# Routing tables, start-up loads and code placement in a fused attention and two-layer mixture-of-experts kernel

## The reference

```python
def _attn_ref(r, k, v, w, u):            # batch 4, 8 heads, 768 steps, head size 48
    for t in range(S):
        kt, vt, rt = k[:, :, t], v[:, :, t], r[:, :, t]
        cur = einsum('bhd,bhe->bhde', u[None] * kt, vt)
        y[:, :, t] = einsum('bhd,bhde->bhe', rt, state + cur)
        state = w[None, :, :, None] * state + einsum('bhd,bhe->bhde', kt, vt)

def _moe_ref(x, w_skip, w_gate, w1, w2): # 3072 rows of 384, 8 experts, hidden size 1024
    do = x @ w_skip > 0
    e, gate = argmax(x @ w_gate), its softmax value
    return x + where(do, gate * (relu(x @ w1[e]) @ w2[e]), 0)

def _moe2_ref(x, w_gate, w1, w2):        # the same without skip and residual
    return gate * (relu(x @ w1[e]) @ w2[e])
```

## Time and profile before

| | us |
|---|---|
| median of 3 runs | 594.66 (594.61 to 594.92) |
| the profiled execution's own time | 589.84 |
| its span | 588.1 |
| TensorE busy | 539.8 (92%) |
| VectorE busy | 387.9 (66%) |
| ScalarE busy | 251.9 (43%) |
| GpSimd busy | 249.9 (42%) |
| mean granted TensorE clock | 0.971 |

### The profile page before, as it was taken

How to read it: one execution, slowest core, us unless ns; L and a number is a source line. 1 busy time by engine, 2 the same in 40 slices (tenths; PEclk the granted TensorE clock), 3 DMA queues, 4 the chain that set the end, 5 groups by cost and what they waited for, 6 DMA issues and landing times. The chain is left out here.

```text
span 588.1 us, 16050 instructions
## 1 busy us (share of the span) xinstructions
PE 539.8 (92%) x5550; PEld 512.8 (87%) x5551; DVE 387.9 (66%) x839; ACT 251.9 (43%) x704; POOL 249.9 (42%) x348
## 2 busy tenths in 40 slices
PE   3999999988799999999857879999999999999992
PEld 3899998978699999999855769999999999999992
DVE  5888888867688878888613927463747464647330
ACT  0233333334077667776413017362736352626220
POOL 5887778742244444454410043232534323324331
PEclk9999999997899999999969989999999999999997
DMA  9798888876187777776378014544444534111100
GB/s 140 121 188 165 161 161 162 169 254 224 43 312 223 209 230 250 244 236 212 60 245 304 0 54 115 185 157 147 139 165 153 162 140 147 50 46 43 39 15 26
DMA packets 114127, 89.58 MB, mean 152 GB/s; under 512 B 80672, under 2 KB 104931, under 8 KB 114080
## 3 DMA queue, kind: packets, MB, share of 16 engines
q1 hardware_dynamic: 106304, 74.16, 45.1%
q0 software_dynamic: 7776, 14.82, 9.1%
HBM read 80.44 MB, written 13.27 MB: 159 GB/s over the span
## 5 line engine op out<-in xcount | busy, mean ns | idle before, releaser
L822 DVE TENSOR_TENSOR w_lo<-w_raw,w_hi 128x384 fp32r<-128x384 f32 (+1 forms) x224 | 130.2, 608 | 4.7 <-ACT w_hi L817 3.1
L1092 PE MATMUL e_ps_h<-e_x_hi,w_hi 128*128 128x192 f32 (+3 forms) x384 | 119.6, 311 | 3.2 <-DVE e_x_lo L1210 2.9
L817 ACT CAST w_hi<-w_raw 128x384 fp32r<-128x384 f32 (+1 forms) x224 | 119.9, 566 | 3.8 <-issue 3.5
L1094 PE MATMUL e_ps_h<-e_x_hi,w_lo 128*128 128x192 f32 (+3 forms) x384 | 119.6, 311 | 0.0
L1093 PE MATMUL e_ps_h<-e_x_lo,w_hi 128*128 128x192 f32 (+3 forms) x384 | 119.5, 311 | 0.0
L1250 DVE SCALAR_TENSOR_TENSOR e_h_lo<-e_ps_h,e_h_hi 128x128 fp32r<-128x128 f32 (+1 forms) x192 | 70.5, 396 | 44.5 <-ACT e_h_hi L1179 40.1
L1092 PE MATMUL e_ps_y<-w_hi,e_h_hi 128*128 128x384 f32 x272 | 95.5, 351 | 0.0
L1094 PE MATMUL e_ps_y<-w_hi,e_h_lo 128*128 128x384 f32 x272 | 91.5, 336 | 0.0
L1093 PE MATMUL e_ps_y<-w_lo,e_h_hi 128*128 128x384 f32 x272 | 91.1, 335 | 0.0
L1092 PEld LDWEIGHTS e_ps_h<-e_x_hi,w_hi 128*128 128x128 f32 x384 | 72.9, 190 | 5.4 <-DVE e_x_lo L1210 3.4
L1094 PEld LDWEIGHTS e_ps_h<-e_x_hi,w_lo 128*128 128x128 f32 x384 | 72.9, 190 | 1.2
(11 more groups left out here) (168 smaller groups left out, 922.4 us busy)
## 6 DMA issues: line engine op xcount, KB each, us to landing
w_raw<-in_moe_w_dram SPq DMA_DIRECT2D x32, 1536.0 KB, 7.3
r_in<-in_r_dram SPq DMA_DIRECT2D x24, 192.0 KB, 3.2
k_in<-in_k_dram SPq DMA_DIRECT2D x24, 192.0 KB, 3.9
v_in<-in_v_dram SPq DMA_DIRECT2D x24, 192.0 KB, 4.0
x_rows<-rows SPq DMA_DIRECT2D x24, 192.0 KB, 3.5
w_lo<-x_rows SPq DMA_DIRECT2D x6, 768.0 KB, 6.6
x_in<-x_rows,e_ent_in POOLq DMA_INDIRECT x33, 3.1
out_dram<-y_rows,e_ent_out POOLq DMA_INDIRECT x19
```

Of the source, the lines that this page charges most:

```text
L817: act.copy(self._of(self.hi1[par], self.hi2[par], n), self._of(self.raw1[par], self.raw2[par], n)).then_inc(self.hi_done[par], 1)
L822: eng.tensor_tensor(self._of(self.lo1[par], self.lo2[par], n), self._of(self.raw1[par], self.raw2[par], n), self._of(self.hi1[par], self.h ...
L1092: pe.matmul(o, s_hi, m_hi, start=(k == 0), stop=False)
L1094: return pe.matmul(o, s_lo, m_hi, start=False, stop=(k == last))
```

## The change

1. Attention's head: w is loaded straight into `w_pow[:, 0]`, by ScalarE's queue, as is u; VectorE waits for w alone. SP begins with r and k at once. GpSimd zeroes only the padding columns. `shrink` is no longer a reciprocal: GpSimd builds it in a ladder of seven multiplies while VectorE builds `grow`. `shrink_up` is made after the first `rk`, and turned by TensorE after the scores of step 0. Loads of r, k and of v get semaphores of their own.
2. Routing: the place is split into row and column in float; instead of 14 wide VectorE instructions there are, for each of the 24 tiles, one for `col_hot` (38 or 45 columns, ids only) and one for `row_hot` (128 columns), both with per-partition scalars, so the placing product has half the columns and its result is copied by one instruction.
3. Experts' head: 24 `gate_hot` instructions on VectorE, 24 products `row_hot` x `gate_hot` on TensorE ahead of `stay_warm`, which has two turns instead of three, and a copy to `gates`; the m = 0 pieces of W.lo come behind that copy.
4. `load_rows` starts two DMAs of half the size.
5. For m = 1, ScalarE's and VectorE's routing programs stand in a one-trip loop whose head is placed at slot 0 of a block of 256 instructions.
6. The wait for the last scatter of m = 1 goes from GpSimd to SP. A smaller edit: the iota that the chain needs has its own semaphore.

```diff
 # attention: SP, GpSimd, ScalarE, VectorE, TensorE
-            sp.wait_ge(dve_zeroed, 2)
-            for j in range(2):
-                sp.dma_start(w_col[PAD * j:PAD * j + D, :], ...).then_inc(small, 16)
-            sp.dma_start(u_row[:], ...).then_inc(small, 16)
...
-                pool.memset(r_in[n][:], 0.0).then_inc(zeroed, 1)
-                pool.memset(k_in[n][:], 0.0).then_inc(zeroed, 1)
+                pool.memset(r_in[n][:, :, D:PAD], 0.0).then_inc(zeroed, 1)
+                pool.memset(k_in[n][:, :, D:PAD], 0.0).then_inc(zeroed, 1)
...
+            pool.memset(shrink[:, :, HALF - 1:HALF], 1.0).then_inc(shrunk, 1)
+            for n in range(6):
+                m = 2 ** n
+                pool.wait_ge(shrunk, n + 1)
+                pool.wait_ge(tables, POWERS[n])
+                pool.tensor_tensor(shrink[:, :, HALF - 2 * m:HALF - m], shrink[:, :, HALF - m:HALF], w_pow[:, n, :]..., ALU.mult).then_inc(shrunk, 1)
+            pool.wait_ge(shrunk, 7)
+            pool.wait_ge(tables, LOW)
+            pool.tensor_tensor(shrink[:, :, HALF:P], shrink[:, :, 0:HALF], grow[:, :, 0:1]..., ALU.mult).then_inc(shrunk, 1)
...
+            act.wait_ge(dve_zeroed, 1)
+            for j in range(2):
+                act.dma_start(w_pow[PAD * j:PAD * j + D, 0, :], ...).then_inc(w_loaded, 16)
+            act.dma_start(u_row[:], ...).then_inc(u_loaded, 16)
...
-            dve.wait_ge(small, 48)
-            link(dve.tensor_copy(w_pow[:, 0, :], w_col[:]))
+            dve.wait_ge(w_loaded, 32)
...
-            link(dve.reciprocal(shrink[:, :, 0:P // 2], grow[:, :, 1:P // 2 + 1]))
-            link(dve.tensor_tensor(shrink[:, :, P // 2:P], ...))
-            link(dve.tensor_tensor(shrink_up[:], ...))
...
+            dve.wait_ge(shrunk, 8)
             rk(0, 0)
+            dve.tensor_tensor(shrink_up[:], ...).then_inc(tables, 1)
...
-                pe.wait_ge(loaded[b], 48 * (c + sub // 4 + 1))
+                pe.wait_ge(rk_loaded[b], 32 * (c + sub // 4 + 1))
...
                 ins.then_inc(scored, 1)
+                if isinstance(i, int) and i == 0:
+                    pe.wait_ge(tables, TABLE_STEPS + 1)
+                    for p in range(NP):
+                        ins = pe.transpose(ps_x[:, P * p:P * p + P], shrink_up[:, p, :], ident[:])
+                    ins.then_inc(tab_ps, 1)
...
                 wait(pe, state_done, i)
+                pe.wait_ge(v_loaded[b], 16 * (c0 + sub0 // 4 + 1))
                 pe.wait_ge(k_end_done, i + 1)
 # load_rows
-    eng.dma_start(dst, x_rows.rearrange(...)[g]).then_inc(x_loaded[g], 16)
+    for n in range(2):
+        eng.dma_start(dst[:, half * n:half * n + half, :], src[:, half * n:half * n + half, :]).then_inc(x_loaded[2 * g + n], 16)
 # route
+        def from_line_start(eng):
+            return nc.Fori(0, 1, engines=[eng.engine], head_slot={eng.engine: 0}) if TURN else nullcontext()
...
-            dve.wait_ge(made, 7)
+                dve.wait_ge(e_made, 1)
...
-            link(dve.tensor_scalar(slot_i[:], slot[:], -1.0, None, ALU.add))
-            link(dve.tensor_scalar(row_i[:], slot_i[:], P - 1, None, ALU.bitwise_and))
-            link(dve.tensor_scalar(col_i[:], slot_i[:], 7, None, ALU.logical_shift_right))
-            for n in range(2):
...
+                link(dve.tensor_scalar(slot_at[:], slot[:], -HALF_UP, 1.0 / P, ALU.add, ALU.mult))
+                link(dve.tensor_scalar(col[:], slot_at[:], ROUND, -ROUND, ALU.add, ALU.add))
+                link(dve.scalar_tensor_tensor(row[:], col[:], -float(P), slot[:], ALU.mult, ALU.add))
+                for place in range(PLACES):
+                    for i in range(GP * place, GP * place + GP):
+                        dve.tensor_scalar(col_hot[:, i, :], col_iota, col[:, i:i + 1], ids[:, i:i + 1], ALU.is_equal, ALU.mult)
+                        ins = dve.tensor_scalar(row_hot[:, i, :], row_iota[:], row[:, i:i + 1], None, ALU.is_equal)
+                    ins.then_inc(hots_ready, 1)
...
-                    ins = pe.matmul(ps_placed, row_hot[:, i, :], placing[:, 2 * NCOL * i:2 * NCOL * (i + 1)], ...)
+                    ins = pe.matmul(ps_placed, row_hot[:, i, :].bitcast(F32), col_hot[:, i, :], ...)
...
-            dve.tensor_copy(table[:, 0:NCOL, 1].bitcast(F32), ps_table[:, 1, :])
 # moe: SP, GpSimd, TensorE, VectorE
+            end = sp.value_load(starts[0:1, E:E + 1], min_val=1, max_val=top)
+            sp.wait_ge(scattered, 16 * (end + 1))
             if m == 0:
                 load_next(sp)
+            else:
+                sp.sem_inc(all_stored, 1)
...
-            end = pool.value_load(starts[0:1, E:E + 1], min_val=1, max_val=top)
-            if m == 1:
-                pool.wait_ge(scattered, 16 * (end + 1))
...
-            stay_warm(pe, ident, ps_y[0][:, 0:P], 3)
+            for i in range(TILES):
+                pe.wait_ge(gates_hot, i + 1)
+                ins = pe.matmul(ps_y[1][:, 0:USED], row_hot[:, i, :].bitcast(F32), gate_hot[:, i, :], start=(i == 0), stop=(i == TILES - 1))
+            ins.then_inc(gates_placed, 1)
+            stay_warm(pe, ident, ps_y[0][:, 0:P], WARM)
...
             start_spans(dve)
+            for i in range(TILES):
+                dve.tensor_scalar(gate_hot[:, i, :], col_iota[:, 0:USED], col[:, i:i + 1], gate[:, i:i + 1], ALU.is_equal, ALU.mult).then_inc(gates_hot, 1)
+            dve.wait_ge(gates_placed, 1)
+            dve.tensor_copy(gates[:, 0:USED], ps_y[1][:, 0:USED]).then_inc(gates_out, 1)
...
-                gate = table[:, bass.ds(t + n, 1), 1:2].rearrange("p o w -> p (o w)").bitcast(F32)
-                dve.tensor_scalar(y_rows[n][:], ps_y[n % 2][:, 0:D], gate, None, ALU.mult).then_inc(y_done, 1)
+                dve.tensor_scalar(y_rows[n][:], ps_y[n % 2][:, 0:D], gates[:, bass.ds(t + n, 1)], None, ALU.mult).then_inc(y_done, 1)
```

More of the change, by code:

```diff
@@ L1 @@
-from contextlib import ExitStack
+from contextlib import ExitStack, nullcontext
 import concourse.bass as bass
@@ L39, in attention @@
     HD = H * D
-    TABLE_STEPS = 20
+    HALF = P // 2
+    POWERS = [1, 1, 2, 3, 4, 5]
+    LOW = 8
+    TABLE_STEPS = 16
     G = lg.shape[2]
@@ L373, in _ @@
             stay_warm(pe, ident, ps_a[0][:, 0, :], 2)
-            pe.wait_ge(tables, TABLE_STEPS)
-            for p in range(NP):
-                ins = pe.transpose(ps_x[:, P * p:P * p + P], shrink_up[:, p, :], ident[:])
-            ins.then_inc(tab_ps, 1)
             def step(c, sub):
@@ L500, in route @@
         slot = sb("slot", [P, TILES])
-        slot_i = sb("slot_i", [P, TILES], I32)
-        row_i = sb("row_i", [P, TILES], I32)
-        col_i = sb("col_i", [P, TILES], I32)
-        entry = sb("entry", [P, TILES, 2])
-        row_iota = sb("row_iota", [P, P], I32)
-        row_hot = sb("row_hot", [P, TILES, P])
-        placing = sb("placing", [P, TILES * 2 * NCOL])
-        col_hot = placing[:].rearrange("p (i w c) -> p i w c", w=2, c=NCOL)
-        col_is = sb("col_is", [P, TILES // 2, NCOL])
+        slot_at = sb("slot_at", [P, TILES])
+        ids = sb("ids", [P, TILES])
+        col_hot = sb("col_hot", [P, TILES, NCOL])
+        row_hot, gate, row, col, row_iota, col_iota = hots
         if TURN:
-            xT = [sb("xT", [P, GRP, CH, P])[:], placing[:, 0:GRP * CH * P].rearrange("p (b c t) -> p b c t", b=GRP, c=CH)]
+            xT = [row_tiles[GRP * n:GRP * n + GRP] for n in range(2)]
             lT = sb("lT", [P, P])
@@ L591, in _ @@
             if not TURN:
[L592 to L594 removed]
+                for row_tile in fresh_rows:
+                    pool.memset(row_tile[:], 0.0).then_inc(made, 1)
+                pool.memset(table[:, NCOL:table.shape[1]], NOWHERE).then_inc(made, 1)
                 pool.wait_ge(made, 8 + len(fresh_rows))
@@ L720, in _ @@
-            count = seen[:, :, TILES - 1:TILES].to_broadcast([P, E, LIMITS])
-            dve.wait_ge(limits_made, 3 if m == 0 else 6)
-            link(dve.tensor_tensor(over[:], count, limit[:].unsqueeze(1).to_broadcast([P, E, LIMITS]), ALU.is_gt))
-            link(dve.tensor_reduce(n_tiles[:], over[:], AX.X, ALU.add))
-            link(dve.tensor_tensor_scan(tiles_incl[:], keep[:, 0, 1:1 + E], n_tiles[:], 0.0, ALU.mult, ALU.add))
-            link(dve.tensor_tensor(base[:], tiles_incl[:], n_tiles[:], ALU.subtract))
@@ L748, in _ @@
-            if not TURN:
-                for n in range(W.N1 // 2):
-                    W.lo(dve, 0, 0, n)
-            if m == 0:
-                link(dve.tensor_tensor(over_short[:], seen[:, :, TILES - 1:TILES].to_broadcast([P, E, MOST]), short_limit[:].unsqueeze(1).to_broadcast([P, E, MOST]), ALU.is_gt))
-                link(dve.tensor_reduce(full[:], over_short[:], AX.X, ALU.add))
-                dve.scalar_tensor_tensor(starts[:, E + 2:2 * E + 2], full[:], float(TALL), base[:], ALU.mult, ALU.add)
-            else:
-                link(dve.tensor_tensor(over[:], over[:], of_full[:].unsqueeze(1).to_broadcast([P, E, LIMITS]), ALU.mult))
```

(12 more changed lines are left out.)

241 lines of the change are left out of this document (129 added, 112 removed).

## The result

The kernel after takes 611.86 us (median; 609.32 to 613.59), beside 594.63 us for the kernel before: 1.0288 of it, 95% interval 1.0247 to 1.0329. So it is 17 us slower, where 3.5 us were predicted, and outside the range. The profiled execution of after took 612.87 us (span 611.1), that of before 589.84 (span 588.1), so the traces differ by 23 us, 6 more than the medians. The executions of the kernel before that were timed beside the experiments lie between 590.13 and 598.09 us, so its trace, at 589.84, is a lucky one: faster than all of them. The trace of after is 1 us slower than its median.

What follows compares the result with a forecast made beforehand. TensorE, busy 92% of the span, was taken to bound the loops, with edits only where it waits or idles. The terms -1.3 + 0.6 + 4.6 + 1.1 - 3.8 - 0.1 + 4.6 - 2.2 = +3.5 on 594.66 gave 598.2 us, range 593.0 to 602.2.

Steps and rivals of the forecast that it cites:

- Steps 3 and 7: Experts' heads, first and second layer: 40 more TensorE instructions at 0.114 in the full clock, +4.6 us each.
- Step 2 and 6: Placing, first and second routing: small one-hots on VectorE at 0.35 a pair, +0.6 and -0.1 us.
- Step 4: Loads between the layers: eight half-size issues at about 0.45 instead of four, +1.1 us (bounds +0.5 and +2.4).
- Step 5: Second routing: ScalarE's 4.78-us pause goes with the program at the head of a block, -3.8 us (bounds -3.8 and 0).
- rival (b): Second routing: ScalarE's pause isn't removed, or an equal one comes elsewhere, +3.8, 602.0 us; chance 0.16.
- Step 1: Attention's head: the loops start 1.4 us earlier, of which -1.3 us is kept (bounds 0 and -3).
- Rival (d): Attention's first `rk`: attention moves by all that VectorE gains, loops 6.5 earlier, -1.7, 593.0 us; chance 0.12.
- Step 8: The end: GpSimd's last drain starts at 580.3, no longer waiting for the scatter, -2.2 us (bounds -2.8 and 0).
- (c): Placing, both routings: small instructions are cheap (0.22), terms fall to -1.0 and -1.5, 595.2 us, no difference; chance 0.17.
- (e): Experts' heads: a product costs by its moving columns, so each head adds 1.5, not 4.6; 592.0 us; chance 0.05.

Runs made afterwards that it cites:

- run 1: Kernel after with the moving side of the 24 gate products read three times over (114 and 135 columns): 602.16 us, ratio 1.0154.
- run 4: Kernel before with the 24 idle turns of each experts' head as plain products of 38 and 45 columns: 606.66 us, ratio 1.0182.
- run 5: Kernel before with the 24 idle turns of each experts' head as 24 plain products of 128 columns (48 instructions): 596.15 us, ratio 1.0023.
- run 2: Kernel after with the 16 idle turns of each experts' head moved ahead of the gate products: 611.3 us, ratio 1.0315.
- run 8: Kernel before with attention's head, programs at the head of a line and the end's wait on SyncE alone: 588.07 us, again 587.36.
- run 11: Kernel of run 8 with the four transposes of `shrink_up` ahead of turning step 1: 584.7 us, ratio 0.9838.
- run 7: Kernel before with only the second routing's loads halved: 595.89 us, ratio 1.0031.
- run 9: Kernel before with attention's head and the end's wait on SyncE, without the programs at the head of a line: 591.2 us, ratio 0.9956.
- run 10: Kernel after without the jump to the head of a line: 616.08 us, ratio 1.0338.

## Why the prediction was wrong, and where it was right

**Steps 3 and 7, the experts' heads, are the error**: +20 instead of +9.2. The step read "that stretch is as long with products in it as with transposes, so the 40 instructions more fall into the full clock: 40 x 0.114". The number of instructions and 0.114 were right (run 1: +4.66 for the first head). The stretch at 1.2 GHz did not stay as long as it had been: it lasted through all 48, and through the turns behind them (runs 1, 4 and 5). The rows that I rested on were of products at full clock with 76 and 90 columns, and of the clock's return under 128-column turns; no row showed a return under 38 columns, and I carried one over to the other without a bound. No rival had the clock in it, so the range could not hold the result. The Trainium skill (TensorE: Matmul & The Clock Gate, "Part 1: The HAM clock gate") says that the gate goes by how busy TensorE has been. By that the clock should have risen; the rows of after and of runs 2 and 4, busy without a gap at 0.50, disagree, and in runs 1 and 5 it did rise under as many instructions, made wide. Both heads together cost 10.7 us more than forecast, of the 19.5 by which the traces' difference exceeds it (13.7 by the medians).

**Step 2 and 6, placing**: +2.3 and +1.9, predicted +0.6 and -0.1. The pair of one-hots cost 0.41, where I took 0.35, worked out from a row of 384 columns with one pointer scalar, and had 0.44 as the upper bound. The bound held, the value was too low. `row_hot` was right, 0.20 from start to start; `col_hot`, 38 columns and two pointer scalars, takes 0.21, not 0.15. That is 1.5 us per route; the rest of the second is TensorE's low clock in its last products.

**Step 4, the loads**: +1.9 to +2.1, predicted +1.1. The mechanism was right; the issues took 0.56 each, not 0.45, inside the bounds.

**Step 5, ScalarE's pause**: -1.8 (run 8: -2.7 and -2.8), predicted -3.8. The pause did go, and from the first copy to the chain the gain is 3.9, as forecast. But I wrote that the jump "may have to be fetched ... but the first copy is not due until 4.5 us after the barrier", and priced it at nothing; from the jump to the first copy it took 6.5 us in after, 5.7 in run 8, and the first copies came 2.2 and 1.3 us later than before. That is the mechanism of rival (b), an equal pause elsewhere, at half its price or less. The Trainium skill (Runtime: NRT & Kernel Launch, "Instruction fetch mechanics") calls the crossing into the next block mostly hidden. Here pauses of 4.6 to 5.2 us come, go and change place with the layout, and 5.4 to 6.9 us pass from a jump to the first copy (nine traces). That they are fetches fits all of this, the instruction packets in each of them above all; no row says which engine a packet serves, and what makes some fetches long stays open.

**Step 1, attention's head**: +0.6 in the trace of after, predicted -1.3. VectorE was ready at 10.3 instead of 15.2, and `k_end` came only 0.66 earlier (15.95): the queue behind it held the gain back, as the step said, but it came 0.75 later than my 15.2; TensorE began to turn step 1 at 12.2, not 11.7, and the rest is in the path behind it. All steps kept their 0.7 until the last one, where TensorE has a pause in the middle of its last products, 0.85 us before and 1.40 after, with no releaser:

```profile
129.67 0.26 PE L433 MATMUL ps_y<-v_in,scoresT 128*64 128x48 f32 x2 [1.40 <-issue]
```

and the clock fell earlier than before, into the last logits. Of nine more executions with this head, seven have attention 0.1 to 0.8 shorter than the trace of before and two 0.9 and 1.1 longer; three without it are 0.2 to 0.9 longer. So the head gives some 0.5, and +0.6 was one execution's share of what varies. What failed is the step from "the loops start 1.4 earlier" to the whole: in run 8 they start 1.6 earlier, and most of it is lost again at attention's end. Rival (d) falls, and run 11 shows what stood against it; its own start of 8.7 doesn't follow from its terms either (9.3 less the 1.4 of blocked links is 7.9).

**Step 8, the end**: -2.3, predicted -2.2, with the drain as long as before.

**The rivals.** (c) fell, since small instructions weren't cheap. (e) fell: at full clock 38 columns take about the time of 76 (24 instructions in 2.77 us in run 1's placing). It was right that columns matter to TensorE, but through the clock, which it didn't name, and with the opposite sign.

## What to carry to other kernels

When a product's moving side gets narrower, look at the granted clock of its stretch, not at the engine's busy share: here fewer columns at the same count cost some 10 us, and reading the same columns three times over won it back. Before pricing work at the full clock, find a row in which work of that shape raised it; if there is none, the price at 1.2 GHz belongs in the range. And when a change consists of several parts, run the good ones alone: three parts of this change and one reordering are 1.6% faster than the kernel before, while the part that gave it its name cost the most.

## What the runs showed that I had not expected

- TensorE stayed at 1.2 GHz through 10.3 us of gapless products of 38 and 45 columns, and fell back to it within such products after it had risen (run 2).
- Pauses of 4.6 to 5.2 us without a releaser in straight-line code of ScalarE and VectorE, whose place and existence hang on the layout (before, runs 4, 5, 7, 9 and 10), each with an instruction packet inside it, and 5.4 to 6.9 us from a jump to the first copy.
- VectorE's `tensor_scalar` with two pointer scalars takes 0.30 us for 38 or 45 columns, and with one 0.27 for 128 columns; how much of it is the pointers wasn't tried.
- GpSimd's drain behind its last scatter takes 5.4 us whether it starts 0.9 or 3.2 us behind the start of the issue.
